# The first pair's q and k of a pooled and local attention: two ways to bring them in and turn them

## The reference, cut to what matters

```python
q_d = q.reshape(B, H, Sd, 4, D).mean(axis=3)          # pooled by four: 144 tokens; k_d, v_d alike
out_d = softmax(q_d @ k_d.T / sqrt(D)) @ v_d          # repeated four times along the tokens
mask = np.abs(pos[:, None] - pos[None, :]) < 4        # local attention in a band
out = out_up + softmax(where(mask, q @ k.T / sqrt(D), -1e9)) @ v
x = moe(x, w_in, w_out)                               # 512 -> 2048, ELU, -> 512
return moe2(x, domain_probs, w1, w2)                  # four experts 512 -> 1024 -> 512, gated sum
```

## Time and profile before

| what | value |
|---|---|
| time, median of three runs | 649.97 us (649.82 to 650.29) |
| the profiled execution: its time, its span | 650.72 us, 648.9 us |
| PE busy | 639.9 us, 99% of the span |
| DVE, ACT, POOL busy | 345.6, 285.7, 322.5 us (53%, 44%, 50%) |
| chain that ended last | PE 94%, ACT 2%, DVE 2% |
| DMA | 46.13 MB, mean 71 GB/s |

### The profile page before, as it was taken

One profiled execution on the slowest core, in us unless ns is written; L12 is line 12 of the kernel. 1 busy time (PEld: TensorE's weight loads), 2 busy tenths in 40 slices (PEclk: granted clock), 3 DMA queues, 4 the chain that ended last, 5 costly groups with the idle time before them and its releaser, 6 DMA issues.

```text
span 648.9 us, 13048 instructions
## 1 busy us (share of the span) xinstructions
PE 639.9 (99%) x4746; PEld 593.5 (91%) x4746; DVE 345.6 (53%) x764; ACT 285.7 (44%) x778; POOL 322.5 (50%) x278
## 2 busy tenths in 40 slices
PE   8999999999999999999999999999999999999998
PEld 5789999999999999998898899899899899889986
DVE  5866454545457787764553454454355255265342
ACT  4878474747385685563133142152052152142210
POOL 3674535353498799889337138047055064160200
PEclk9999999999999999999999999999999999999999
DMA  9945424241113112303003002011011011010012
GB/s 187 246 99 146 127 80 126 80 104 65 66 66 130 65 66 71 124 1 116 16 2 130 0 25 105 0 65 65 0 65 65 0 65 65 1 66 1 1 49 97
DMA packets 51491, 46.13 MB, mean 71 GB/s; under 512 B 31616, under 2 KB 33920, under 8 KB 51456
## 3 DMA queue, kind: packets, MB, share of 16 engines
q1 hardware_dynamic: 51456, 45.67, 23.4%
HBM read 43.30 MB, written 2.36 MB: 70 GB/s over the span
## 4 chain that ended last, share of the span: by engine, by line
PE 94%; ACT 2%; DVE 2%; issue 0%; DVEq 0%; ACTq 0%
PE psum L513 16%; PE psum L515 16%; PE psum L514 16%; PE psum L585 11%; PE psum L587 11%; PE psum L589 11%; PE psum L655 2%; PE psum L654 2%; PE psum L653 2%; PE psum L505 1%; PE psum L431 1%; PE psum L445 1%; PE psum L499 1%; PE psum L460 1%; PE psum L389 1%; PE psum L480 1%
## 5 line engine op out<-in xcount | busy, mean ns | idle before, releaser
L1615 POOL TENSOR_TENSOR wb_lo<-wb_raw,wb_hi 128x512 fp32r<-128x512 f32 x64 | 81.7, 1292 | 183.1 <-ACT wb_hi L899 183.1
L1425 DVE SCALAR_TENSOR_TENSOR o_acc<-psum,gate_now,o_acc 128x512 f32<-128x512 f32 x72 | 54.0, 750 | 127.1 <-PE psum L515 127.0
L515 PE MATMUL psum<-wb_hi,h_lo 128*128 128x512 f32 x288 | 112.3, 390 | 0.0
L514 PE MATMUL psum<-wb_lo,h_hi 128*128 128x512 f32 x288 | 112.2, 390 | 0.0
L513 PE MATMUL psum<-wb_hi,h_hi 128*128 128x512 f32 x288 | 112.0, 389 | 0.0
L1009 ACT ACTIVATE h_hi<-psum 128x320 fp32r<-128x320 f32 (+1 forms) x128 | 52.4, 411 | 87.4 <-DVE psum L1397 40.3
L1615 POOL TENSOR_TENSOR wa_lo<-wa_raw,wa_hi 128x512 fp32r<-128x512 f32 x60 | 77.5, 1317 | 16.9 <-ACT wa_hi L940 16.9
L1015 ACT COPY sums<-psum 128x256 f32<-128x256 f32 (+1 forms) x32 | 12.8, 400 | 155.1 <-PE psum L589 155.1
L589 PE MATMUL psum<-x_hi,wa_lo 128*128 128x256 f32 (+2 forms) x228 | 67.4, 296 | 0.0
L587 PE MATMUL psum<-x_lo,wa_hi 128*128 128x256 f32 (+2 forms) x228 | 67.3, 295 | 0.0
L585 PE MATMUL psum<-x_hi,wa_hi 128*128 128x256 f32 (+2 forms) x228 | 67.2, 295 | 0.0
(11 more groups left out here) (194 smaller groups left out, 1680.8 us busy)
## 6 DMA issues: line engine op xcount, KB each, us to landing
wa_raw<-in_moe_w_in SPq DMA_DIRECT2D x8, 1024.0 KB, 5.5
wb_raw<-in_moe_w_out SPq DMA_DIRECT2D x8, 1024.0 KB, 5.1
wa_raw<-in_moe_w SPq DMA_DIRECT2D x8, 1024.0 KB, 4.9
wb_raw<-in_moe_w SPq DMA_DIRECT2D x8, 1024.0 KB, 5.0
out<-o_acc SPq DMA_DIRECT2D x9, 256.0 KB, 2.0
q_in<-in_q SPq DMA_DIRECT2D x10, 144.0 KB, 4.6
k_in<-in_k SPq DMA_DIRECT2D x10, 144.0 KB, 4.6
v_in<-in_v SPq DMA_DIRECT2D x5, 288.0 KB
```

The lines of the kernel that those rows point to most:

```text
L514: nc.tensor.matmul(bank_cols, w_hi(n), x_lo_(n), start=False, stop=False)
L515: last = nc.tensor.matmul(bank_cols, w_lo(n), x_hi_(n), start=False, stop=(n == chunks - 1))
L1425: nc.vector.scalar_tensor_tensor(o_acc[:, m, :], psum[:, DOWN2_BANKS[(MT * half + m) % 2], :], gate_now[:, m:m + 1], o_acc[:, m, :], ALU.m ...
L1615: nc.gpsimd.tensor_tensor(lo[:, c, :], raw[:, c, :], hi[:, c, :].bitcast(F32), ALU.subtract).then_inc(lo_ready, 1)
```

## The change

Pair 0's q and k are loaded and turned in another way, and pooled at another place:
- Loading: one DMA for q and one for k (instead of two each), with eight neighbouring tokens in each of 72 partitions, so that a piece in memory is 2,048 bytes. The set needs more room along a row, so pair 0 now uses the set in `o_acc` and pair 1 the own set (`held` gives 1, 0, 2, 3). SP's waits ahead of pair 4's loads become `qk_used(1)` and `v_used(1)`.
- Turning: for each of the eight tokens of a partition and each head one ordinary product of 72 by 64 with the identity (16 for q, 16 for k, in place of 6 transposes each). In PSUM the tokens then lie in the order a, r, p, where token = 8p + 4a + r.
- Pooled sums: DVE takes q's and k's from PSUM, over r, which lies 72 elements apart; q is unscaled in them, and the scale 1/8 goes into pair 0's exponential. The copies `copy_first_qT` (ACT) and `take_first_kT` (DVE) come after these sums, wait for them, and write with a step of eight elements to bring the tokens into order.
- Fills: 7 and 3 instead of 9 and 5.

```diff
+RUN, RUNS = 8, SEQ // 8
-FILL_INPUTS, FILL_SUMS = 9, 5
+FILL_INPUTS, FILL_SUMS = 7, 3
...
+    q_first = q[0, 0:2].rearrange("h (p c) d -> p h (c d)", c=RUN)
+    k_first = k[0, 0:2].rearrange("h (p c) d -> p h (c d)", c=RUN)
...
+        def turned(first, order):
+            return psum[:, first:first + 2, 0:HALF].rearrange(f"q a (r p) -> {order}", r=FACTOR)
+        def by_token(t):
+            return t.rearrange("q (p a r) -> q a r p", a=2, r=FACTOR)
...
-            return u if isinstance(u, int) and u < HALF_PAIRS else 0
+            return (1, 0, 2, 3)[u] if isinstance(u, int) and u < HALF_PAIRS else 0
+        def pooled_scale(u):
+            return (HD ** -0.5 if isinstance(u, int) and u == 0 else 1.0) / FACTOR ** 2
...
+            def load_first():
+                for src, dst, loaded in ((q_first, q_in[held(0)], q_loaded), (k_first, k_in[held(0)], k_loaded)):
+                    sp.dma_start(dst, src).then_inc(loaded[held(0)], 16)
...
-            load_qk(0)
+            load_first()
...
-            qk_used(0)
+            qk_used(1)
             load_qk(HALF_PAIRS)
-            v_used(0)
+            v_used(1)
...
+            def turn_first(loaded, source, first, done):
+                pe.wait_ge(loaded[held(0)], 16)
+                for c in range(RUN):
+                    for h in range(2):
+                        last = nc.tensor.matmul(psum[HD * h:HD * (h + 1), first + c // 4, RUNS * (c % 4):RUNS * (c % 4 + 1)],
+                                                source[held(0)][:, h, HD * c:HD * (c + 1)], ident[0:RUNS, 0:RUNS],
+                                                start=True, stop=True)
+                last.then_inc(done, 1)
...
-            turn_q(0)
-            turn_k(0)
+            turn_first(q_loaded, q_in, IN_BANKS[ALONE][0], q_turned)
+            turn_first(k_loaded, k_in, IN_BANKS[ALONE][1], k_turned)
...
+            def copy_first_qT():
+                act.wait_ge(qTs_ready, 1)
+                nc.scalar.activation(by_token(qT[0]), turned(IN_BANKS[ALONE][0], "q a r p"), ACT.Copy,
+                                     scale=HD ** -0.5).then_inc(qT_copied, 1)
...
-            copy_qT(0, ALONE)
+            copy_first_qT()
...
+            def take_first_sums(banks, turned_in, sums_, ready):
+                dve.wait_ge(turned_in, 1)
+                nc.vector.tensor_reduce(sums_[0][:, 0:POOLED].rearrange("q (p a) -> q a p", a=2), turned(banks, "q a p r"),
+                                        X, ALU.add).then_inc(ready, 1)
+            def take_first_kT():
+                dve.wait_ge(kTs_ready, 1)
+                nc.vector.tensor_copy(by_token(kT[0]), turned(IN_BANKS[ALONE][1], "q a r p")).then_inc(kT_copied, 1)
...
-            take_qTs(0)
-            take_first_kTs()
-            take_kT(0)
+            take_first_sums(IN_BANKS[ALONE][0], q_turned, qTs, qTs_ready)
+            take_first_sums(IN_BANKS[ALONE][1], k_turned, kTs, kTs_ready)
+            take_first_kT()
```

More of the change, by code:

```diff
@@ L152, in program, with input_set @@
         qk_size, v_size = NLT * 2 * HD, 4 * FACTOR * HD
-        def input_set(spare):
+        FIRST_SIZE = RUN * 2 * HD
+        def input_set(spare, qk_size=qk_size):
             k_at, v_at, win_at = qk_size, 2 * qk_size, 2 * qk_size + v_size
+            if qk_size == FIRST_SIZE:
+                return (spare[0:RUNS, 0:k_at].rearrange("p (h n) -> p h n", h=2),
+                        spare[0:RUNS, k_at:v_at].rearrange("p (h n) -> p h n", h=2),
+                        spare[0:PT, v_at:win_at].rearrange("p (a n) -> p a n", a=4),
+                        spare[0:WIN, win_at:win_at + NQT * 2 * HD].rearrange("p (c h d) -> p c h d", h=2, d=HD))
             return (spare[0:LT, 0:k_at].rearrange("p (c n) -> p c n", c=NLT),
@@ L164, in program @@
                   h_spare2[:].rearrange("p f n -> p (f n)"))
-        q_in, k_in, v_in, v_win = zip(own_set, *(input_set(spare) for spare in spares))
+        q_in, k_in, v_in, v_win = zip(own_set, input_set(spares[0], FIRST_SIZE), *(input_set(spare) for spare in spares[1:]))
         v_sum, v_part = [sb1("v_sum0", [PT, 4, HD]), sb1("v_sum1", [PT, 4, HD])], sb1("v_part", [PT, 4, HD])
@@ L860, in exponentiate @@
                     act.wait_ge(attn_turned, 4 * (u - 1) + (1, 2, 4)[j])
-                out, width, scale = (attn_p, POOLED, 1.0 / FACTOR ** 2) if j == 0 else (attn, WIN, 1.0)
+                out, width, scale = (attn_p, POOLED, pooled_scale(u)) if j == 0 else (attn, WIN, 1.0)
                 c0, c1 = SPANS[j] if j else (0, NPQ)
@@ L1204, in row_max @@
                     dve.wait_ge(max_p_ready, u + 1)
-                    nc.vector.tensor_scalar(neg_max[:, STATS[0]], neg_max[:, STATS[0]], 1.0 / FACTOR ** 2, None,
+                    nc.vector.tensor_scalar(neg_max[:, STATS[0]], neg_max[:, STATS[0]], pooled_scale(u), None,
                                             ALU.mult).then_inc(max_ready, 1)
```

## The result

The change made the kernel slower. Over 22 executions of each, the median is 653.20 us (650.04 to 653.44) against 650.47 us (649.70 to 650.88); the ratio of the means is 1.0024, with a 95% interval of 1.0013 to 1.0035. I had forecast 648.7 us, in a range of 647.9 to 650.2.

The account below looks back on a forecast made before the run. The start-up chain to the first scores sets when PE's fixed dense block from 43.4 us begins. Fills 0.83, minus 0.3 for turning, plus 0.76 for the copy give 1.29 us off 649.97: 648.7 us, range 647.9 to 650.2.

Parts of the forecast that it names:

- Bound, and how a shift is carried: Behind 43.4 us PE is busy without a gap; a gain in the first microseconds arrives whole if it survives until then.
- Loads: Start: q lands at 3.9 to 4.1 us, k at 4.7 to 5.4; PE asks at 4.19 and 5.2; cost nothing.
- Turning: q's 16 products take 1.3 us, done at about 5.5, costing 0.3 at the lower clock; k's done at 6.1.
- given back on the way: Gain partly lost before 43.4 us, by product halves not overlapping (1.0 of 1.3 gone) or another hand-over; 649.3 us, chance 0.12.
- Sums: Pooled sums straight from PSUM take ScalarE's copy of q off the chain before the first scores; plus 0.76 us.
- price of steps: Strided PSUM reads by the sums and SBUF writes by the copies cost nothing; upper end 0.75 us more for either sum.
- Pair 4's k: Lands at 37.6 us, when PE, shifted by 1.3, would ask for it; costs 0.1 us at most.
- The clock: TensorE rises from 1.2 to 2.4 GHz at about 5.7 us, within q's turning or right after it.
- the clock rises late: TensorE's lower level lasts to about 13 us; 3.1 us cost less 1.3 won, 1.8 slower, 651.8 us; chance 0.06.

Follow-up runs that it names:

- the sums with eight and with seven fills: Kernel before with q's pooled sums from PSUM and eight fills (median 649.94 us) or seven fills (six at 649.75 to 650.13, five at 651.26 to 651.95).
- lower group: Faster of the two groups of executions; changed kernel without further edit: ten of 22 around 650.3 us.
- only the sums: Kernel before with q's pooled sums taken from PSUM ahead of ScalarE's copy, nine and five fills: median 650.23 us beside 650.58, ratio 0.9994.
- only the fills: Kernel before with seven and three fills instead of nine and five: median 649.99 us beside 650.58, ratio 0.9998.
- upper group: Executions above 652.5 us; changed kernel without further edit: twelve of 22 around 653.3 us.

## Why the prediction was wrong

**Bound, and how a shift is carried.** Right. The dense run behind 43.4 us is the same in both kernels, and a first score earlier by some tenths ends the kernel earlier by as many (640.3 to 640.4 in the table). It held with 0.7 us won (before with seven and three fills). With 0.9 and 1.1 won (the sums with eight and with seven fills) pair 4's k was 1.0 us late in both profiles.

**Loads.** Wrong: the term that I put at nothing. I had q at 3.9 to 4.1 and k at 4.7 to 5.4; q's products started at 4.3 to 4.8 in the five profiles with five or seven fills, k's at 5.96 and 5.68 in the lower group. The pieces of 2 KB brought no faster rate (over 2 to 4 us 218 and 230 GB/s in the changed kernel's two profiles, 232 before). k's load also shared the engines with pair 1's, which SP now issued 1 us sooner: held back, k had landed 0.3 to 0.5 us earlier. q's load was to be covered by the fills and cost 0.3; k's was to be covered by q's turning and went onto the chain.

**Turning.** Wrong by a factor. I read the 36 records of the earlier trace rows as 36 products; they are 18, since each fp32 product is two records. So 16 products take 1.22 us at 2.4 GHz, not 0.7, and 2.1 at 1.2 GHz, not 1.3. A transpose is one record: six took 0.66 to 0.71 at 2.4 GHz and about 1.2 at 1.2 GHz. The step that I costed at +0.3 was worth +0.5 at the upper level and +0.9 at the lower one.

**What these two cost in the lower group.** The first scores' product of zeros came at 8.13, not 7.12: k's products started at 5.96 instead of 5.2 and ended at 7.2 instead of 6.1, so that DVE stood still for 0.59 us ahead of its sum of k, and 1.0 of the 1.29 us was gone. The rival "given back on the way" had just this (k at about 7.2, scores at about 8.1, 1.0 of 1.3 gone), but from products that are slow at the lower level; here they ran at the upper one and k landed late. The agreement of its numbers is luck.

**Sums.** Right as to their length, 0.76 us each from PSUM, and ScalarE's copy is off the chain. The 0.76 us won by that did not arrive whole, though: in the kernel before alone it was 0.35, since k's turning comes next. The price of steps, which I set at nothing for all four operations, is nothing for the two sums' reads and 0.44 and 0.57 us for the two copies' writes. The Trainium skill (SBUF — State Buffer, "Door 1: The DMA port swizzle") states a penalty for touching a new 16-byte line with each element. For writes the runs agree and give it a size, about six to nine tenths of the copy's own time (0.44 on 0.76, 0.57 on 0.65). The same section of the Trainium skill calls any non-contiguous PSUM access slow for matmuls. For VectorE's read no run here shows a cost.

**Pair 4's k.** Wrong as a bound. I took its issue at 29.48 as fixed and its slack as 1.2 us. In the changed kernel it was issued 1.4 us later (29.03 to 34.3 instead of 27.64 to 32.6) and landed at about 38.0, 0.6 us ahead of its use, and in two kernels that gained more at the start it was 1.0 us late. In two kernels whose loads are those of the kernel before (only the sums, only the fills) the issue also began 0.8 and 0.7 us later than there, so part of the delay needs no change of the loads. Why SP's queue runs later stays open.

**The clock.** This is the step that made the kernel slower and not only no faster. For the forecast I had said that the clock rises at about 5.7 us as before: it rose at about 4 us in the two profiles of the lower group, and at about 12.7 in that of the upper one, the group of twelve of the 22 executions. The rival "the clock rises late" had its place and its sum right: I wrote that the lower level would last to about 13 us and cost 3.1 us gross; the profile shows 12.7 us and 3.2 us between the spans. The terms of that sum were not right. I had 0.4 for k's turning, where both turnings cost 1.6 (each product is two records), and 1.2 for work behind pair 1's q, where the clock was up again; that the two errors cancel is luck. The condition was wrong, and with it the chance of 0.06. Not a pause keeps the clock down: TensorE was busy 11.44 of 11.50 us and stayed at 1.2 GHz. Two things moved the share of late rises: the number of fills ahead (5 of 5 executions with five, 16 of 34 with seven, 3 of 34 with eight to eleven), and the kind of product behind them. With transposes and seven fills there is only a group about 1 us late, of which it isn't shown whether the clock makes it.

The Trainium skill (TensorE: Matmul & The Clock Gate, "Part 4: PE-mode transpose") says that transposes don't count as busy for the clock. I took that as a reason for less risk with ordinary products. The runs show the reverse for these tiles: four of eleven executions with ordinary products in the upper group, none of 33 with transposes.

What I could not see from one profile is the spread. One profiled execution of the kernel before shows one moment of rise. Its times spread over 1.2 us with the same instructions, and that was a hint. The profile of the kernel with only the order of the loads changed, whose start is that of the kernel before, agrees: there the clock rises later within the turnings (k's take 0.80 us instead of 0.66) and the first scores come 0.14 us later. That the rise makes the whole spread is likely but not shown. Outside the upper group the profiles of the experiments show it between about 4 and 7 us.

## What to carry to other kernels

Fills ahead of the first real products are no filler: count them as the price of the clock, and after taking any out, time the kernel often enough to see whether its times split in groups. Don't put ordinary fp32 products in the place of transposes in a start-up chain, and find out how many records a product leaves before you divide the duration of a row by their number. When a start-up chain is shortened, look up the next load that its end will ask for, with the slack of each; here 1.2 us of slack were gone when 0.9 us had been won.

## What the runs showed of the hardware that I had not expected

- TensorE can be busy 99% of 11 us and stay at 1.2 GHz, when seven wide fills are followed by small fp32 products (72 by 64 with 72 columns, 64 by 64 with 144). The changed kernel with the same products, in other executions, is at 2.4 GHz from 4.4 us on. With seven fills 16 of 34 executions were late, with nine and eleven 1 of 22.
- A wait of 1.0 us at 38 us was followed by a granted clock of 0.63 over 4 us in one kernel (PE had waited 0.37 us shortly before), while a wait of 0.95 us at the same place in another left it at 1.00.
- A step of 32 bytes in SBUF makes a ScalarE copy of 576 elements 1.22 instead of 0.65 us and a VectorE copy 1.20 instead of 0.76; reading PSUM 288 bytes apart costs VectorE nothing (0.76 and 0.75).
- Loads in 2 KB pieces over 72 partitions, with pair 1's loads held back so that nothing else moved, went at 211 and 244 GB/s from 2 to 3 and 3 to 4 us, hardly faster than 256-byte pieces over 96 partitions (228 and 235), with a DMA share of 0.73 and 0.81 instead of 0.99 and 1.04. The weights, 2 KB pieces over 128 partitions, reached 382 GB/s.
